# Reordering the hand-over from the dense stage to the expert slots of a fused attention and mixture-of-experts kernel

## The reference, cut to what matters

```python
x = ((x @ w1) * (x @ w2)) @ w3 @ w_out            # dense stage
logits = x @ w_gate + modality_bias[modality_id]  # 8 logits for a token
e_idx = np.argmax(logits, axis=1)
gate_w = softmax(logits)[np.arange(N), e_idx]
for e in range(8):
    mask = e_idx == e
    out[mask] = gate_w[mask, None] * (relu(x[mask] @ ew1[e]) @ ew2[e])
```

## Time and profile before

| | |
|---|---|
| median of 3 runs | 996.33 us (995.99 to 996.59) |
| the profiled execution | 998.51 us |
| its span, first to last instruction | 996.5 us |
| TensorE busy | 943.0 us, 95% of the span |
| mean granted TensorE clock | 0.981 of full speed |
| VectorE, ScalarE, GpSimd busy | 446.8, 312.5, 260.8 us |

### The profile page before, as it was taken

One profiled execution on the slowest core, in us unless ns is written; L12 is line 12 of the kernel. 1 busy time (PEld: TensorE's weight loads), 2 busy tenths in 40 slices (PEclk: granted clock), 3 DMA queues, 4 the chain that ended last, 5 costly groups with the idle time before them and its releaser, 6 DMA issues.

```text
span 996.5 us, 19721 instructions
## 1 busy us (share of the span) xinstructions
PE 943.0 (95%) x6562; PEld 848.4 (85%) x6563; DVE 446.8 (45%) x1233; ACT 312.5 (31%) x850; POOL 260.8 (26%) x336
## 2 busy tenths in 40 slices
PE   2999999999999999999999979988999999999996
PEld 1778799989999989999899979977888888888885
DVE  6564665554664564564556542344222222222221
ACT  3343533343343343333333422211222222222221
POOL 3450111132212231221222222463630004620000
PEclk9899999999999999999999989998999999999998
DMA  5563022223133222222222203137111115111110
GB/s 167 151 201 117 22 54 65 61 65 107 32 87 93 64 65 65 64 75 72 64 75 54 64 33 139 60 131 243 55 42 42 42 42 210 42 42 42 42 42 23
DMA packets 106749, 78.73 MB, mean 79 GB/s; under 512 B 85295, under 2 KB 85295, under 8 KB 106672
## 3 DMA queue, kind: packets, MB, share of 16 engines
q1 hardware_dynamic: 102432, 64.06, 22.8%
q0 software_dynamic: 4240, 13.66, 3.6%
HBM read 56.44 MB, written 21.53 MB: 78 GB/s over the span
## 4 chain that ended last, share of the span: by engine, by line
PE 84%; DVE 6%; issue 5%; POOL 2%; ACT 1%; DMA 0%; SPq 0%; POOLq 0%; DVEq 0%; ACTq 0%
PE acc_a L308 5%; PE acc_a L310 5%; PE acc_a L309 5%; PE attn L308 5%; PE attn L310 5%; PE attn L309 5%; PE acc_b L308 4%; PE acc_b L310 4%; PE acc_b L309 4%; PE attn L917 4%; PE acc_a L314 4%; PE acc_b L314 4%; PE acc_b L316 3%; PE acc_b L315 3%; PE acc_a L316 3%
## 5 line engine op out<-in xcount | busy, mean ns | idle before, releaser
L737 POOL TENSOR_TENSOR probs<-scores,row_inv 128x256 f32<-128x256 f32 x96 | 68.6, 736 | 267.0 <-DVE row_inv L1686 267.0
L314 PE MATMUL acc_b<-xT_w,w 128*128 128x384 f32 x256 | 89.6, 350 | 3.2 <-DVE ab L1737 3.2
L314 PE MATMUL acc_a<-xT_w,w 128*128 128x384 f32 x256 | 90.2, 352 | 0.9 <-ACT row_third L1267 0.9
L316 PE MATMUL acc_a<-xT_w,w 128*128 128x384 f32 x256 | 86.6, 338 | 0.0
L316 PE MATMUL acc_b<-xT_w,w 128*128 128x384 f32 x256 | 86.6, 338 | 0.0
L315 PE MATMUL acc_b<-xT_w,w 128*128 128x384 f32 x256 | 86.5, 338 | 0.0
L315 PE MATMUL acc_a<-xT_w,w 128*128 128x384 f32 x256 | 86.4, 338 | 0.0
L1288 ACT ACTIVATE scores<-scores,neg_max 128x136 f32<-128x136 f32 x192 | 75.7, 397 | 26.9 <-DVE neg_max L1676 26.9
L308 PE MATMUL attn<-bufs,uT_hi 128*128 (+1 forms) x200 | 80.3, 401 | 0.0
L310 PE MATMUL attn<-bufs,uT_lo 128*128 (+1 forms) x200 | 78.1, 391 | 0.0
L309 PE MATMUL attn<-bufs,uT_hi 128*128 (+1 forms) x200 | 78.0, 390 | 0.0
(11 more groups left out here) (321 smaller groups left out, 2566.6 us busy)
## 6 DMA issues: line engine op xcount, KB each, us to landing
raw<-in_moe_w SPq DMA_DIRECT2D x40, 512.0 KB, 5.9
x_in<-routed SPq DMA_DIRECT2D x28, 257.0 KB, 3.0
q_nat<-in_q SPq DMA_DIRECT2D x24, 256.0 KB, 3.2
k_nat<-in_k SPq DMA_DIRECT2D x24, 256.0 KB, 4.0
v_nat<-in_v SPq DMA_DIRECT2D x24, 256.0 KB, 4.2
x_mid<-x_out SPq DMA_DIRECT2D x24, 256.0 KB, 2.0
x_in<-x_mid SPq DMA_DIRECT2D x24, 256.0 KB, 2.7
raw<-in_moe_w_out SPq DMA_DIRECT2D x4, 512.0 KB, 5.6
```

Source lines behind the costliest of these rows:

```text
L314: pe.matmul(o, w_hi, x_hi, start=start, stop=False, skip_group_check=True)
L316: return pe.matmul(o, w_lo, x_hi, start=False, stop=stop, skip_group_check=True)
L737: pool.tensor_tensor(probs[:, at, side * HALF:(side + 1) * HALF], scores[:, at, side, SINKS:], row_inv[:, at].unsqueeze(2).broadcast_to([P ...
```

## The change: five orders and two waits

The products are the same, and so are the loops from slot 2 on. What is moved or added:

1. `count(first_full, ...)` goes from behind `mlp_a(6, 7)` to behind `mlp_b(6, 4)` on TensorE, and `first_expert()` from behind the `mlp_x` of two tiles to behind `mlp_uT(6, 5)` on VectorE.
2. The first quarter of `slot_h(0, 1, 0)` is put before the last `route_rank`, and the other three behind it; on VectorE `take_gates(0)` goes behind `route_choice` and `route_place`.
3. `slot_hT(0)` goes before `slot_h(1, 1, 0)` on TensorE and ScalarE; on VectorE `slot_X_lo(1)` and `take_gates(1)` go into the tables, ahead of some ten operations that make `rows_known`, and `slot_hT(0)` right behind `rows_known`.
4. `slot_x(2, 0, 2)` is put in the middle of `slot_y(0, 1)`.
5. SyncE writes the padding behind the first expert's region first (one transfer more than before, with a semaphore of its own, `pad_sent_first`). After the paddings of the even experts are issued it waits for that one and for the scattered rows, and loads slot 2's rows from an address that needs no table. GpSimd waits for `pad_sent_first` before it issues the paddings of the odd experts.

```diff
--- before.py
+++ after.py
@@ -244,7 +244,7 @@
         zeroed, relation, sides = sem("zeroed"), sem("relation"), sem("sides")
         flag_known, masks_ready, tables_ready, bias_ready = map(sem, ("flag_known", "masks_ready", "tables_ready", "bias_ready"))
         rows_known, slots_known = sem("rows_known"), sem("slots_known")
-        pad_ready, pad_sent, pad_sent_odd = map(sem, ("pad_ready", "pad_sent", "pad_sent_odd"))
+        pad_ready, pad_sent, pad_sent_odd, pad_sent_first = map(sem, ("pad_ready", "pad_sent", "pad_sent_odd", "pad_sent_first"))
         expert_in = sems("expert_in", CHUNKS)
         split_hi = sem("split_hi")
         slot_in = sems("slot_in", 2)
@@ -619,13 +619,19 @@
             sp.wait_ge(pad_ready, 2)
             sp.dma_start(routed[PAD_ROW:PAD_ROW + P, :], padding[:, :]).then_inc(pad_sent, 16)
             sp.wait_ge(ends_known, 1)
+            end = sp.value_load(ends_i[0:1, bass.ds(first, 1)], min_val=0, max_val=PAD_ROW - P)
+            sp.dma_start(routed[bass.ds(end, P), :], padding[:, :]).then_inc(pad_sent_first, 16)
             for e in range(0, E, 2):
                 end = sp.value_load(ends_i[0:1, e:e + 1], min_val=0, max_val=PAD_ROW - P)
                 sp.dma_start(routed[bass.ds(end, P), :], padding[:, :]).then_inc(pad_sent, 16)
+            sp.wait_ge(pad_sent_first, 16)
+            for r in row_sent:
+                sp.wait_ge(r, TILES // GT * 16)
+            sp.wait_ge(X_full, 1)
+            sp.wait_ge(gates_done, 1)
+            sp.dma_start(x_in[:, 0, :], routed[bass.ds(first * REGION + 2 * P, P), :]).then_inc(slot_in[0], 16)
             sp.wait_ge(pad_sent, (E // 2 + 1) * 16)
             sp.wait_ge(pad_sent_odd, E // 2 * 16)
-            for r in row_sent:
-                sp.wait_ge(r, TILES // GT * 16)
             sp.wait_ge(rows_known, 1)
 
             def load_slot(t, par):
@@ -656,10 +662,10 @@
                 next_slot(t + 3, 1 - par)
                 next_expert(t)
 
-            next_slot(2, 0)
+            next_slot(3, 1)
             sp.wait_ge(slots_known, 1)
             n_slots = sp.value_load(misc_i[0:1, 0:1], min_val=1, max_val=SLOTS - 1)
-            slot(0, 0)
+            next_expert(0)
             slot(1, 1)
             with sp.Fori(0, TILES // 2 - 1) as j:
                 for odd in (2, 3):
@@ -804,6 +810,7 @@
                 send_row(group_tile(GROUPS - 1, j))
             pool.wait_ge(pad_ready, 2)
             pool.wait_ge(ends_known, 1)
+            pool.wait_ge(pad_sent_first, 16)
             for e in range(1, E, 2):
                 end = pool.value_load(ends_i[0:1, e:e + 1], min_val=0, max_val=PAD_ROW - P)
                 pool.dma_start(routed[bass.ds(end, P), :], padding[:, :]).then_inc(pad_sent_odd, 16)
@@ -1048,17 +1055,18 @@
                     mm = pe.transpose(left[:, c * P:(c + 1) * P], x_in[:, par, c * P:(c + 1) * P], ident[:, :])
                 mm.then_inc(X_full, 1)
 
-            def slot_h(t, buf, half):
+            def slot_h(t, buf, half, chunks=range(KD)):
 
                 o, taken, full = ((acc_a, h0_taken, h0_full), (acc_b, h1_taken, h1_full))[half]
                 if half == 0:
                     pe.wait_ge(X_lo, t + 1)
                 pe.wait_ge(taken, t)
-                for c in range(KD):
+                for c in chunks:
                     at = c * FE + half * 512
                     hi, lo = (bufs[:, bass.ds(buf, 1), part, at:at + 512].rearrange("p a n -> p (a n)") for part in (0, 1))
                     mm = triple(pe, o[:, :], xT_hi[:, c, :], xT_lo[:, c, :], hi, lo, c == 0, c == KD - 1)
-                mm.then_inc(full, 1)
+                if KD - 1 in chunks:
+                    mm.then_inc(full, 1)
 
             def slot_hT(t):
                 pe.wait_ge(h0_taken, t + 1)
@@ -1070,16 +1078,17 @@
                         mm = pe.transpose(o[:, c * P:(c + 1) * P], u[:, at:at + P], ident[:, :])
                     mm.then_inc(hT_full, 1)
 
-            def slot_y(t, buf):
+            def slot_y(t, buf, chunks=range(KF)):
 
                 pe.wait_ge(y_done, t)
-                for c in range(KF):
+                for c in chunks:
                     if c % 4 == 0:
                         pe.wait_ge(hT_lo, 2 * t + 1 + c // 4)
                     at = c * DM
                     hi, lo = (bufs[:, bass.ds(buf, 1), part, at:at + DM].rearrange("p a n -> p (a n)") for part in (2, 3))
                     mm = triple(pe, attn[:, :], uT_hi[:, c, :], uT_lo[:, c, :], hi, lo, c == 0, c == KF - 1)
-                mm.then_inc(y_full, 1)
+                if KF - 1 in chunks:
+                    mm.then_inc(y_full, 1)
 
             def weights_of(t):
 
@@ -1179,6 +1188,8 @@
                 attn_scores(tb)
                 mlp_a(g, 4)
                 mlp_b(g, 4)
+                if g == GROUPS - 2:
+                    count(first_full, GROUPS - 2)
                 mlp_a(g, 5)
                 mlp_b(g, 5)
                 attn_probsT(tb)
@@ -1189,8 +1200,6 @@
                 attn_values(tb)
                 attn_scores(tc)
                 mlp_a(g, 7)
-                if g == GROUPS - 2:
-                    count(first_full, GROUPS - 2)
                 mlp_b(g, 7)
                 for quarter in range(4):
                     mlp_x2(g, 0, 0, quarter)
@@ -1219,21 +1228,23 @@
             mlp_x2(g, 2, 0, 0, 1, 2, 3)
             slot_x(0, 0, 1)
             mlp_x2(g, 2, 1, 0, 1, 2, 3)
+
+            pe.wait_ge(w_split, SPLIT_W + KD)
+            slot_h(0, 1, 0, (0,))
             route_rank(g)
-
-            pe.wait_ge(w_split, SPLIT_W + KD)
-            slot_h(0, 1, 0)
+            slot_h(0, 1, 0, (1, 2, 3))
             count(count_full, GROUPS)
             pe.wait_ge(x2_taken, 2 * TILES)
             slot_h(0, 1, 1)
             slot_x(1, 1, 1)
+            slot_hT(0)
             slot_h(1, 1, 0)
-            slot_hT(0)
             slot_h(1, 1, 1)
             pe.wait_ge(w_split, SPLIT_W + CHUNKS)
-            slot_y(0, 1)
-
+            slot_y(0, 1, range(4))
             slot_x(2, 0, 2)
+            slot_y(0, 1, range(4, KF))
+
             slot_h(2, 1, 0)
             slot_hT(1)
             slot_h(2, 1, 1)
@@ -1934,6 +1945,8 @@
                 mlp_uT(g, 4)
                 mlp_u(g, 5)
                 mlp_uT(g, 5)
+                if g == GROUPS - 2:
+                    first_expert()
                 take_probsT(tb, 0)
                 take_probsT(tb, 1)
                 mlp_u(g, 6)
@@ -1946,8 +1959,6 @@
                 sums(tc, 1)
                 mlp_x(ta)
                 mlp_x(tb)
-                if g == GROUPS - 2:
-                    first_expert()
                 take_probsT(tc, 0)
                 take_probsT(tc, 1)
                 after = group_tile(g + 2, 0) if g < GROUPS - 2 else None
@@ -1964,9 +1975,9 @@
             ve.memset(padding[:, 0:DM + 1], 0.0).then_inc(pad_ready, 1)
             ve.memset(padding[:, DM + 1:ROW], float(NO_TOKEN)).then_inc(pad_ready, 1)
             slot_X_lo(0)
-            take_gates(0)
             route_choice(g)
             route_place(g)
+            take_gates(0)
 
 
             ve.wait_ge(count_full, 1)
@@ -2026,6 +2037,8 @@
             op(ve.tensor_reduce(start, pairs_c[:, :, :], AX.X, ALU.add))
             op(ve.tensor_reduce(place_k, pairs_d, AX.X, ALU.add))
             done()
+            slot_X_lo(1)
+            take_gates(1)
 
             op(ve.tensor_tensor(end, start, tiles_of, ALU.add))
             op(ve.tensor_scalar(base, start, -float(P), -float(PAD_ROW), ALU.mult, ALU.add))
@@ -2053,8 +2066,7 @@
             op(ve.tensor_tensor(slot_b[:, :, :], slot_a[:, :, :], inner(place_k, by_slot), ALU.mult))
             done()
             ve.tensor_scalar(rows_i[:, :], f[0], float(PAD_ROW), None, ALU.add).then_inc(rows_known, 1)
-            slot_X_lo(1)
-            take_gates(1)
+            slot_hT(0)
 
             op(ve.tensor_reduce(f[2], slot_b[:, :, :], AX.X, ALU.add))
             done()
```

## The result

The changed kernel took 980.19 us in the median of 4 runs (979.74 to 980.77), the kernel before 996.46 us (995.99 to 998.68). The ratio is 0.9833 with a 95% interval of 0.9816 to 0.9850. The forecast was 978.3 us in a range of 975.7 to 982.7. The profiled executions are 998.51 us before and 980.20 us after, their spans 996.5 and 978.2: 18.3 us apart, where the medians are 16.3 apart. The sum of the prediction was 18.0.

A forecast was written before the change was run, and what follows sets the result against it. TensorE, busy 943.0 of 996.5 us, was taken as the bound, so only its stalls and slow clock could be won. Gains of 7.9 (group 6) and 10.1 (hand-over) made 18.0 us: 978.3 us from the 996.33 median, range 975.7 to 982.7.

The forecast's parts named there:

- The sum: Hand-over: 25.3 us work plus 2.0 stalls, 27.3 in place of 37.4, gaining 10.1; with Part 1, 18.0 us.
- Part 1: Group 6, first expert: wait and slow products behind it go, 8.6 us, less 0.7 at transposes into `right`: 7.9 us.
- rival (e): Group 6: the wait only moves, to the probabilities of `tc`; chance 0.02 with other ways to no gain.
- Rank: Hand-over start: rank at 661.77, 1.87 us after the last dense product, a stall of 1.07 us (bounds 0 and 1.1).
- I take it that the choice is held by the same split: VectorE before the rank: GpSimd's split holds the choice, which ends 0.1 us earlier than before, not 1.3.
- Rival (a): Before the rank: GpSimd's split does not hold small operations with two inputs; time 977.2, chance 0.13.
- I take no: Behind the rank's wait: 1.07 us does not bring the low clock; if it did, 1.6 to 2.0 us more.
- Rival (b): Hand-over: the short waits still bring the low clock, once or in two places; time 980.1 or 982, chance 0.20.
- Slot 0 and slot 1: Hand-over: TensorE stalls 0.54 us before `slot_hT(0)` and 0.41 before `slot_h(1)`; the old 4.83 us wait goes.
- (c): Hand-over: VectorE's spare 0.2 us or the rows of slots 2 and 3 fall short; 979.3 to 982, chance 0.12.
- (d): Middle of `slot_y(0)`: slot 2's rows come very late and hold `slot_x(2)`; slower, 1000.8 if landing at 700, chance 0.03.
- against the median of 996.33 it gives 978.3: Last step: the 18.0 us gain, made in the profiled execution of 998.51 us, is set against the median, giving 978.3.

The follow-up runs named there:

- e1: Kernel before, with only the earlier `count(first_full, ...)` and `first_expert()` added and its hand-over left as it was: 989.11 us, ratio to before 0.9920.
- e2: Changed kernel with `count(first_full, ...)` and `first_expert()` put back in their old places: 988.04 us, against 980.29 for the unaltered changed kernel.
- e3: Changed kernel with `take_gates(0)` put back ahead of `route_choice` and `route_place` on VectorE: 980.39 us, against 980.29 for the unaltered changed kernel.
- e7: Changed kernel with GpSimd's split of the first expert's eighth weight piece made by ScalarE (high part) and VectorE (low part) instead: 978.93 us.
- e4: Changed kernel with the last `route_rank` put back ahead of the whole first half of `slot_h(0)`: 982.63 us.
- e9: Changed kernel with `slot_X_lo(1)` and `take_gates(1)` put back behind `rows_known`, directly ahead of `slot_hT(0)`, on VectorE: 984.65 us.
- e5: Changed kernel with slot 2's rows loaded as before, behind all paddings and `rows_known`: 987.14 us.
- b0: Kernel before, unaltered, run once more for a second trace: that profiled execution took 996.26 us, with a span of 994.3.
- e6: Changed kernel with `first_expert()` two calls later on VectorE, behind `take_probsT` of `tb`: 980.21 us.
- e8: Changed kernel with `first_expert()` behind `take_probsT` of `tb` and the eighth weight piece split by ScalarE and VectorE: 977.76 us, ratio to before 0.9806.
- c2: Changed kernel, unaltered, run again as control of the third batch: 980.55 us.

## Why the prediction was right, step by step

**Part 1.** Right in mechanism and size. Forecast 7.9 us; e1 and e2 measured 7.95 and 7.75. The 42 products took 5.04 us (578.60 to 583.64) where 5.1 was said, nothing else took the wait's place (rival (e) falls), and the price of putting five operations ahead of `take_probsT` was 0.66 us for 0.7.

**Rank.** The step that said "I take it that the choice is held by the same split" is confirmed by the 1.80 us operation, and by e3 and e7. Its size was a little off: the rank came 2.18 us after the last dense product (651.36 to 653.54), not 1.87, because the split ended 0.29 us after that product and not 0.02 before it. The wait was 1.5 us, not 1.07. Rival (a) falls.

**The low clock after this wait.** "I take no" held: 1.00 in all windows of the hand-over, and the products come every 0.23 us. It held in all eight traces with this wait (1.19 to 1.36 us idle). But the bound that it was drawn from, "1.41 did not and 1.79 did", is no bound: the same trace of the kernel before has a wait of 2.07 us at 116.47 with full clock behind it. Rival (b) did not happen here, but e4 shows how near it was: with 0.44 us more of idle the profiled run had it, and by their times two of the other three.

**Slot 0 and slot 1.** Waits of 0.54 and 0.41 us were forecast and are 0.6 (the transposes would follow at 659.1) and 0.4 by distances. e9 shows that the move of `slot_X_lo(1)` is what made it so.

**The tables and the loads.** VectorE was to reach `slot_X_lo(2)` so that TensorE has 0.2 us to spare; it got there in time by about that much (`slot_X_lo(2)` at 671.53, and 0.73 us on from there is 672.26, against 672.53). The rows of slots 2 and 3 were in time by 1.4 and 4.7 us; the bounds for slot 2 were 3.4 us early to 0.5 us late, and 3 us early was reckoned for slot 3. Rivals (c) and (d) did not happen. e5 shows that the loads are where they could have. The new place of `slot_hT(0)` and the halves of `slot_y(0)` were not tried by themselves.

**The sum.** 27.3 us were forecast for the hand-over and 27.6 measured: 0.4 us more in the rank's wait, and 0.2 less in the work, which was put at 25.3. By distances between the two profiles, group 6 gave 13.82 - 5.16 - 0.66 = 8.0 us and the hand-over 37.4 - 27.6 = 9.8, together 17.8 where 18.0 was forecast. The profiled executions are 18.3 apart. The other 0.5 us is not the change: it is the longer slow stretch in the start-up of the first profile. That 18.3 lies so near to 18.0 owes something to it, and so to luck.

**What was off by 1.9 us** is the last step: "against the median of 996.33 it gives 978.3". The sum took out slow-clock time that the profiled execution had, and subtracted it from a median whose executions mostly don't have it: the three runs shown took 996.0 to 996.6, the profiled one 998.5, and that gap of 2.2 us was in sight. By b0 it is 1.1 us in the hand-over and 0.5 behind `misc_i`, 1.6 in all; 0.2 is the difference of 18.0 and 17.8. The gains by medians say the same: parts 2 to 5 gave 8.8 to 9.0 us, where 10.1 was forecast. From the profiled execution, 998.51 - 18.0 = 980.5, against 980.20 profiled and 980.19 in the median. The changed kernel has no half clock in group 6 and the hand-over in any of its three traces, so its profiled execution and its median agree.

## What to carry to other kernels

When the stretches to be removed contain stalls followed by half clock, make the sum from the profiled execution to the end, and don't move it onto a median of runs that is 2 us lower: first ask which of the removed pieces the other runs had. Set a window's clock beside the distance of its products. Where a long instruction of one engine blocks those of another, moving the first blocked instruction away may only block the next one (e3); move the long one (e7). And before tiny operations are put ahead of the work of a bank, look for the nearest place in that engine's stream where it is idle: here it was two calls on, and the wait of 0.66 us was gone.

## What the runs showed of the hardware that was not expected

- A VectorE operation of 128x8 with two inputs in SBUF waits for a GpSimd operation of 128x1024 to end just as one of 128x384 does: 1.80 us in place of 0.23, and 0.23 again when the GpSimd instruction is gone (e7).
- After idle times of 1.76 to 2.12 us TensorE's clock fell in some executions and stayed in others. It fell after 1.76 (e4), 1.79 (before) and 1.82 us (e1), and stayed after 2.10 (b0). The wait at 115 to 116 us, 2.07 to 2.12 us long in all 14 traces, had half clock behind it in five (e2, e6, e7, e8, e9) and full clock in nine, the two of the kernel before and the three of the changed kernel among them. In e6 and in the changed kernel:

```profile
115.13 0.63 PE L1015 MATMUL misc<-ident,row_out 128*128 128x128 f32 x4 [2.08 <-DVE w_fold L1759]
116.00:118.00 2.00, 2.00 (x9) 2.00 (x8) 0.91 (x3) 1.32 (x5) 1.62 (x3) 0.58 0.00 0
```

```profile
115.86 0.63 PE L1015 MATMUL misc<-ident,row_out 128*128 128x128 f32 x4 [2.07 <-DVE w_fold L1759]
116.00:118.00 2.00, 2.00 (x14) 2.00 (x14) 1.20 (x5) 2.00 (x8) 1.53 (x3) 1.00 0.00 0
```

- From group 6 on, the clock was at half behind each wait of 3.21 us and more, and at full behind each of 1.41 us and less, in all 14 traces. In e9, behind 3.21 us, it fell only 1 us after the products had started again. What tells the cases between apart was not found.
- By the distance of its products, TensorE is at the slow pace from its first products to some 31 to 34 us in all 14 traces. The clock of the windows shows half only in five of them (before, c2, e6, e7, e8), and there only from about 20 us on. When the pace rises differs by 3 us between the traces.
